# Attention with q and k handed over features first: rotary in that layout, one transpose of the maxima, rows placed by DMA

## The reference

```python
q_rot, k_rot = (rotate(q), rotate(k))        # x1*cos - x2*sin, x1*sin + x2*cos
scores = scale * np.matmul(q_rot, k_rot.transpose(0, 1, 3, 2))
scores = scores - np.max(scores, axis=-1, keepdims=True)
attn = np.exp(scores)
attn = attn / (np.sum(attn, axis=-1, keepdims=True) + 1e-09)
x = np.matmul(attn, v)                       # then heads side by side: 2304 x 512
h = x @ w_in;  x = (h - np.tanh(h)) @ w_out                          # layer 1
h = x @ w_in2; out = (h * (1 / (1 + np.exp(-1.702 * h)))) @ w_out2   # layer 2
```

## Time and profile before

| | us |
|---|---|
| median of 3 runs | 1189.93 (1188.15 to 1190.78) |
| the profiled execution | 1188.3, its span 1186.5 |
| start to the first score product | 21.0 |
| attention stage, 32 heads | 355.1 |
| the two layers and the end | 810.4 |
| TensorE busy, whole span | 1146.3 (97%) |
| granted TensorE clock | 1.000 throughout |

### The profile page before, as it was taken

One profiled execution on the slowest core, in us unless ns is written; L12 is line 12 of the kernel. 1 busy time (PEld: TensorE's weight loads), 2 busy tenths in 40 slices (PEclk: granted clock), 3 DMA queues, 4 the chain that ended last, 5 costly groups with the idle time before them and its releaser, 6 DMA issues.

```text
span 1186.5 us, 15852 instructions
## 1 busy us (share of the span) xinstructions
PE 1146.3 (97%) x6320; PEld 1051.4 (89%) x6320; DVE 471.2 (40%) x769; ACT 465.6 (39%) x811; POOL 188.9 (16%) x162
## 2 busy tenths in 40 slices
PE   5999999999999999999999999999999999999998
PEld 4788788777778999999999999999999999999997
DVE  6445545555553642333332323446332232323222
ACT  3655655665655532323222222345322222223222
POOL 6346545646501100000000000000000000000000
PEclk9999999999999999999999999999999999999999
DMA  4233344333321520000000000044000001000101
GB/s 112 51 86 79 78 117 138 86 101 91 104 64 56 186 81 27 27 28 27 27 28 27 1 28 27 27 134 133 27 27 22 5 27 28 27 27 1 27 1 27
DMA packets 78920, 65.79 MB, mean 55 GB/s; under 512 B 32256, under 2 KB 66048, under 8 KB 78848
## 3 DMA queue, kind: packets, MB, share of 16 engines
q1 hardware_dynamic: 78848, 64.79, 19.0%
HBM read 45.74 MB, written 14.23 MB: 51 GB/s over the span
## 4 chain that ended last, share of the span: by engine, by line
PE 89%; ACT 4%; DVE 4%; issue 2%; ACTq 0%; DVEq 0%
PE PS L556 34%; PE PS L574 17%; PE PS L571 17%; PE PS L515 10%; PE PS L500 4%; PE PS L503 3%; PE PS L478 3%; ACT k_hl L627 2%; ACT q_hh L633 1%; DVE q_lm L773 1%; DVE k_hl L768 1%; PE PS L467 1%; PE PS L487 1%; ACT q_lm L620 1%; DVE neg_max L762 1%
## 5 line engine op out<-in xcount | busy, mean ns | idle before, releaser
L556 PE MATMUL PS<-x_hi,w_parts 128*128 128x384 f32 x1536 | 423.1, 336 | 0.0
L556 PEld LDWEIGHTS PS<-x_hi,w_parts 128*128 128x128 f32 x1536 | 280.4, 188 | 4.3
L817 DVE TENSOR_TENSOR g_raw<-PS,act_t 128x384 f32<-128x384 f32 x192 | 107.1, 558 | 403.4 <-ACT act_t L688 202.7
L556 PE MATMUL PS<-x_lo,w_parts 128*128 128x384 f32 x768 | 257.2, 335 | 0.0
L571 PE MATMUL PS<-g_hi,w_parts 128*128 128x384 f32 x768 | 210.3, 334 | 0.8 <-DVE g_lo L822 0.8
L574 PE MATMUL PS<-w_parts,g_hi 128*128 128x512 f32 x576 | 195.1, 393 | 1.0 <-DVE y_sb L831 0.8
L515 PE MATMUL PS<-probs,v_one 128*128 128x288 f32 x640 | 181.7, 406 | 0.3 <-ACT pv_sb L616 0.3
L822 DVE TENSOR_TENSOR g_lo<-g_raw,g_hi 128x384 fp32r<-128x384 f32 x192 | 107.3, 559 | 113.6 <-ACT g_hi L695 113.6
L608 ACT ACTIVATE probs<-PS 128x576 f32<-128x576 f32 x160 | 104.2, 651 | 118.6 <-PE PS L503 113.8
L695 ACT ACTIVATE g_hi<-g_raw 128x384 fp32r<-128x384 f32 x192 | 100.8, 525 | 122.5 <-DVE g_raw L817 119.4
L762 DVE TENSOR_REDUCE neg_max<-PS 128x1 f32<-128x576 f32 x160 | 117.7, 754 | 76.9 <-PE PS L478 75.8
(11 more groups left out here) (64 smaller groups left out, 908.2 us busy)
## 6 DMA issues: line engine op xcount, KB each, us to landing
x_raw<-x_scratch SPq DMA_DIRECT2D x12, 768.0 KB, 4.5
raw_w<-moe_w_in_dram SPq DMA_DIRECT2D x32, 256.0 KB, 3.2
raw_w<-moe_w_out_dram SPq DMA_DIRECT2D x32, 256.0 KB, 3.4
k_h<-k_hl SPq DMA_DIRECT2D x16, 288.0 KB, 3.4
inv_wide<-inv_scratch SPq DMA_DIRECT2D x32, 144.0 KB, 3.0
x_scratch<-x_out SPq DMA_DIRECT2D x16, 288.0 KB, 2.4
x_scratch<-y_sb SPq DMA_DIRECT2D x6, 768.0 KB, 3.5
raw_k<-k_dram SPq DMA_DIRECT2D x16, 256.0 KB, 3.1
```

Of the source, the lines that this page charges most:

```text
L556: last = nc.tensor.matmul(h_banks[j % 2], w_parts[j][:, w, c * P:(c + 1) * P], x[par][:, c, :], start=(c == 0 and w == 0 and x is x_hi), s ...
L817: nc.vector.tensor_tensor(g_raw[:, j % 2, :], h_banks[j % 2], act_t[:, j % 2, :], ALU.subtract if m == 0 else ALU.mult).then_inc(g_done, 1)
```

## The change

The host hands over q and k with features first (64 x 576 per head), so that a pair is 128 rows, features of two heads. What follows in the kernel:

- `load` brings a pair's 128 x 576 block by one DMA into `raw`, and the same block again with each 32 rows swapped with their neighbours by four DMAs of 32 rows into `turned`. Rotary is then raw x cos + turned x sin, in place, three full-width operations. `raw` is now read by `keys_hi`, `queries_hi`, `keys_lo` and `queries_lo` directly, so that the next load into it waits for the low parts.
- `keys_across` and `queries_across` are gone, with their ring slots. `k_hl`, `q_hh`, `k_one` (before `k_h1`) and `q_max` (before `q_lm`) have four buffers, one per head; each head's parts are made three heads ahead (`PREPARED`).
- `maxima_across` is one transpose of a 128 x 5 tile. ACT copies the 5 x 128 result to `max_rows`, and SP places it in one row of `q_max` by two DMAs per head (`place_maxima`). The third and fourth matmul of a head's first score tile wait for that (`row_in`).
- The near scores of tiles 1 to 4 stand in the head before, two after each of its first two tiles; that of tile 0 stands a head earlier still, at its end.
- `copy_k` runs per head. `spread_inverse` is cut in two: `store_inverse` is SP's last step of an even head, `spread_inverse` follows the loads of the odd head.
- Positions keep their order, so that v is loaded plainly, and the result leaves by one DMA per unit, and one per tile at the very end.

```diff
-            if ahead and t < TILES - 1:
-                order.append(("M", h + 1, t))
-                if t == TILES - 2:
-                    order.append(("M", h + 1, t + 1))
-        if h % 2 == 0 and h + 2 < NHEADS:
-            order.append(("K", h + 2, 0))
-        if ahead:
-            order.append(("R", h + 1, 0))
+            if ahead and t < 2:
+                order += [("M", h + 1, 2 * t + 1), ("M", h + 1, 2 * t + 2)]
+            if ahead and t == 2:
+                order.append(("R", h + 1, 0))
         if h + 2 < NHEADS:
-            order.append(("Q", h + 2, 0))
+            order.append(("M", h + 2, 0))
+        turned = {t: [sb(f"turned_{t}{j}", [P, SEQ], stack=one_stack) for j in range(2)] for t in "qk"}
+        k_hl = [sb(f"k_hl{j}", [P, PADDED], F32R, one_stack) for j in range(4)]
+        k_one = [sb(f"k_one{j}", [P, PADDED], F32R, one_stack) for j in range(4)]
+        q_hh = [sb(f"q_hh{j}", [P, PADDED], F32R, one_stack) for j in range(4)]
+        q_max = [sb(f"q_max{j}", [P, SEQ], F32R, one_stack) for j in range(4)]
...
-                par = pair % 2
-                heads = src[2 * pair:2 * pair + 2, :, :]
-                sp.dma_start(raw[t][par][:, :, 0:FULL, :],
-                             heads[:, 0:FULL * P, :].rearrange("a (p i) d -> p a (i d)", i=FULL)).then_inc(loaded[t][par], 16)
-                sp.dma_start(raw[t][par][0:TAIL, :, FULL, :],
-                             heads[:, FULL * P:SEQ, :].rearrange("a p d -> p a d")).then_inc(loaded[t][par], 16)
+                par, first = pair % 2, pair * P
+                sp.dma_start(raw[t][par][:, :], src[first:first + P, :]).then_inc(loaded[t][par], 16)
+                for b in range(P // 32):
+                    to, of = slice(32 * b, 32 * b + 32), first + 32 * (b ^ 1)
+                    sp.dma_start(turned[t][par][to, :], src[of:of + 32, :]).then_inc(loaded[t][par], 16)
...
+            def copy_k(h):
+                sp.wait_ge(k_hi_done, h + 1)
+                sp.dma_start(k_one[h % 4][own(h % 2), 0:SEQ].bitcast(F32), k_hl[h % 4][own(h % 2), 0:SEQ].bitcast(F32)).then_inc(k_copied[h % 4], 16)
+
+            def place_maxima(h):
+                row = q_max[h % 4][one_row(h % 2), :].bitcast(F32)
+                sp.wait_ge(row_done, h + 1)
+                sp.dma_start(row[:, 0:FULL * P].rearrange("o (t n) -> o t n", t=FULL),
+                             max_rows[h % 2][0:FULL, :].bitcast(F32)).then_inc(row_in[h % 4], 16)
+                sp.dma_start(row[:, FULL * P:SEQ], max_rows[h % 2][FULL:TILES, 0:TAIL].bitcast(F32)).then_inc(row_in[h % 4], 16)
...
+            def store_inverse(pair):
+                sp.wait_ge(inv_done, pair + 1)
+                sp.dma_start(inv_scratch[pair].rearrange("a (p j) -> (a p) j", j=SEQ // HD), sums[pair % 2][:, :]).then_inc(inv_out, 16)
...
-            for h in range(NHEADS):
-                pair = h // 2
-                if h % 2 == 0:
-                    if pair + 2 < PAIRS:
-                        sp.wait_ge(k_roped, pair + 1)
-                        load("k", k_d, pair + 2)
-                        sp.wait_ge(q_roped, pair + 1)
-                        load("q", q_d, pair + 2)
-                    if h:
-                        fetch_sums(h - 1)
-                    if pair + 1 < PAIRS:
-                        load_v(pair + 1)
-                    if pair >= 2:
-                        store_x(pair - 2)
-                else:
-                    if pair + 1 < PAIRS:
-                        copy_k(pair + 1)
+            copy_k(1)
+            for h in range(-1, NHEADS):
+                pair = (h + 1) // 2
+                if h % 2 and pair + 2 < PAIRS:
+                    sp.wait_ge(k_lo_done, 2 * pair + 2)
+                    load("k", k_d, pair + 2)
+                    sp.wait_ge(q_lo_done, 2 * pair + 2)
+                    load("q", q_d, pair + 2)
+                if h % 2 and h >= 3:
+                    spread_inverse(h // 2 - 1)
+                if h >= 4 and h % 2 == 0:
+                    store_x(h // 2 - 2)
+                if h >= 1:
                     fetch_sums(h - 1)
-                    if pair:
-                        spread_inverse(pair - 1)
+                if h >= 0 and h % 2 == 0 and h // 2 + 1 < PAIRS:
+                    load_v(h // 2 + 1)
+                if h + 1 < NHEADS:
+                    place_maxima(h + 1)
+                if h + PREPARED < NHEADS:
+                    copy_k(h + PREPARED)
+                if h >= 2 and h % 2 == 0:
+                    store_inverse(h // 2 - 1)
...
-                store_tile((UNITS - 1) * UT + tile)
-            sp.wait_ge(y_stored, stored_by(LAYERS * UNITS))
+                row = (UNITS - 1) * UNIT + tile * P
+                sp.dma_start(out[row:row + P, :], y_sb[:, tile, :]).then_inc(y_stored, 16)
+            sp.wait_ge(y_stored, 16 * (n + UT))
...
+                par, at = pair % 2, ((pair - 1) * 2 + "kq".index(t)) * 2 + 1
+                pool.wait_ge(loaded[t][par], (pair // 2 + 1) * 80)
+                nc.gpsimd.tensor_tensor(turned[t][par][:, :], turned[t][par][:, :], sin_sb[:, :], ALU.mult).then_inc(pool_chain, 1)
+                nc.gpsimd.tensor_tensor(raw[t][par][:, :], raw[t][par][:, :], cos_sb[:, :], ALU.mult).then_inc(pool_chain, 1)
+                pool.wait_ge(pool_chain, at + 2)
+                nc.gpsimd.tensor_tensor(raw[t][par][:, :], raw[t][par][:, :], turned[t][par][:, :],
+                                        ALU.add).then_inc(k_roped if t == "k" else q_roped, 1)
 
...
-                slot = slot_columns(slot_of("R", h), PADDED)
-                for i in range(TILES):
-                    last = nc.tensor.transpose(slot[0:1, i * P:(i + 1) * P], neg_max[h % 2][:, i:i + 1], ident[:, :])
-                last.then_inc(r_ready, 1)
+                nc.tensor.transpose(slot_of("R", h)[0:TILES, 0, 0:P], neg_max[h % 2][:, :], ident[:, :]).then_inc(r_ready, 1)
...
+                    pe.wait_ge(k_copied[h % 4], h // 4 * 16 + 16)
+                slot = slot_halves(slot_of("S", h, t))
+                keys, rows = slice(t * P, (t + 1) * P), slice(0, HD + 1 if h % 2 == 0 else P)
+                for b in range(2):
+                    nc.tensor.matmul(slot[:, b, :], k_hl[h % 4][:, keys], q_hh[h % 4][:, b * HALF:(b + 1) * HALF],
+                                     start=True, stop=False)
+                if t == 0:
                     pe.wait_ge(q_lo_done, h + 1)
+                    pe.wait_ge(row_in[h % 4], h // 4 * 32 + 32)
                 for b in range(2):
+                    last = nc.tensor.matmul(slot[:, b, :], k_one[h % 4][rows, keys],
+                                            q_max[h % 4][rows, b * HALF:(b + 1) * HALF], start=False, stop=True)
...
-                    if ahead and t in (2, 3):
-                        near_scores(h + 1, t)
-                    if ahead and t == 3:
-                        near_scores(h + 1, 4)
-                    if t == 4 and h % 2 == 0 and h + 2 < NHEADS:
-                        keys_across((h + 2) // 2)
-                    if t == 4 and ahead:
-                        maxima_across(h + 1)
                     if now and g >= 0:
                         probs_v(g)
-                    if ahead and t in (0, 1):
-                        near_scores(h + 1, t)
+                    if ahead and t < 2:
+                        near_scores(h + 1, 2 * t + 1)
+                        near_scores(h + 1, 2 * t + 2)
+                    if ahead and t == 2:
+                        maxima_across(h + 1)
                 if h + 2 < NHEADS:
-                    queries_across(h + 2)
+                    near_scores(h + 2, 0)
...
+                if h >= 2:
+                    act.wait_ge(row_in[(h - 2) % 4], (h - 2) // 4 * 32 + 32)
+                nc.scalar.activation(max_rows[h % 2][0:TILES, :], slot_of("R", h)[0:TILES, 0, 0:P], ACT.Copy).then_inc(row_done, 1)
...
+                    if t == 2 and 0 <= h + 1 < NHEADS:
+                        row(h + 1)
                     if t == 2 and h in early_x:
                         cut_x(0, 0, 0, early_x[h])
-                    if t == 2 and h in early_w:
+                    if t == 3 and h in early_w:
                         cut_weights(0, early_w[h])
-                if h % 2 == 0 and h + 2 < NHEADS:
-                    keys_hi(h + 2)
-                if 0 <= h + 1 < NHEADS:
-                    row(h + 1)
-                if h % 2 == 0 and h + 2 < NHEADS:
-                    keys_hi(h + 3)
-                if h + 2 < NHEADS:
-                    queries_hi(h + 2)
+                    if h + PREPARED < NHEADS:
+                        if t == 3:
+                            keys_hi(h + PREPARED)
+                        if t == 4:
+                            queries_hi(h + PREPARED)
...
+            for h in range(-PREPARED, NHEADS):
+                for t in range(1, TILES):
                     if 0 <= h + 1 < NHEADS:
                         row_max(h + 1, t)
```

(18 more changed lines are left out.)

238 lines of the change are left out of this document (79 added, 159 removed).

## The result

The changed kernel takes 1207.51 us (median of 4 runs, 1204.84 to 1212.82) against 1189.87 (1188.15 to 1190.78): a ratio of 1.0156, 95% interval 1.0118 to 1.0193. It is slower by 17.6 us; 1201 had been forecast, in a range of 1176 to 1223. The profiled execution took 1208.82, its span is 1207.0. One of the four runs, 1212.82, had a mean granted clock of 0.933 where the other three had 0.981 to 0.984; it left no trace, and the interval on the median is some 4.5 us to either side.

What follows compares the result with a forecast made beforehand. TensorE bounds the kernel (busy 97%); SP's queue would lengthen pairs. 13.4 + 4.3 + 3 - 2 - 2.8 - 2.8 - 1.8 = +11.3 us: 1199.6 profiled, 1201 median, range 1176 to 1223.

Steps and rivals of the forecast that it cites:

- TensorE's work alone: Attention pair: transposes and a wait of 0.8 go, two transposes come back, 22.27 to 19.2 us.
- The chain through ACT and DVE: Odd head: near tile 2 waits 0.8 for DVE's maximum; head 9.8 to 10.1 us, pair 20.2 by this alone.
- SP's queue: Issues ahead of the even head's maxima make TensorE wait 3.9 us per pair; pair 23.4, +1.1.
- I take 0.60 plus the gap: SP's queue: assumed issue time of a 32-row load, 8 per pair, with no row for it; lower bound 0.43.
- rival (A): Cheap issues on SP: eight small loads at 0.45 to 0.48 each, pair 22.1, time 1183; chance 0.16.
- the prediction's own sign: SP's timeline after the change: turned loads issuing in under 0.5 would show the forecast of 0.6 each wrong.
- its clock is granted in full: TensorE before the change: clock read as 2.4 GHz in both layers and attention; no clock term in the sum.
- Weight issues at head 14: SP behind head 14: eight weight issues at 0.5 delay the next head's placement once, +4.3 us.
- The start: Before and in head 0: more issues, GpSimd passes and queries_hi(2); head 0 longer by 2, start 0 to 1.6 later, +3.
- Last heads: End of attention: no loads left in SP's queue, -2.8 us.
- End: End of kernel: three stores instead of six let the last be issued some 1.8 earlier, -1.8 us.
- The quoted rule that issuing is a small part of a transfer: Skill page on DMA issue, about 50 ns dispatch: queue would cost nothing, pair 20.2, time 1160; rival's chance 0.12.

Runs made afterwards that it cites:

- e7: Changed kernel with ten loads behind the placement, maximum and reciprocal ahead of the queries' low part, weight issues spread over heads 14 to 17: 1161.73 us.
- e8: e7 plus v's loads behind the placement in even heads and GpSimd's first rotary waiting for DVE's first low part: 1151.66 us.
- e5: Changed kernel with GpSimd's first rotary waiting until DVE has finished the first query's low part: 1203.99 us.
- e3: Changed kernel with one of k's four small turned loads cut in two from pair 2 on, same bytes: 1213.94 us.
- e1: Changed kernel with the ten loads of q and k in odd heads moved behind the maxima's placement and the keys' copy: 1185.04 us.

## Why the prediction came out right, and where it was wrong

The sign, the size within 7 us, and the place of the largest loss were right. The terms were less so.

1. **TensorE's work alone: 19.2 per pair. Too high.** The 19.2 that e7 and e8 take in heads 4 to 13 look like it, but hold waits in every odd head (0.4 to 1.4). Without a wait a head takes 8.95 (e8), a pair 17.9. The sum took the work of before as the pair's length less one wait of 0.8. In the even head of before TensorE also stands still twice between the first product with v and the second score tile, which from start to start take 1.08 and 0.82 there against 0.75 and 0.48 elsewhere (the second of these waits is a row of the timeline):

```profile
133.91 0.51 PE L500 MATMUL PS<-q_hh,k_hl 128*128 128x288 f32 x2 [0.33 <-DVE q_lm L773]
```

These 0.7 were not taken off; the other 0.6 I can't place. The forecast didn't hang on it, since the chain of point 2 was the longer one. The change does on TensorE what it says; without the queue it would have been faster than before.
2. **The chain through ACT and DVE: odd head 9.8 to 10.1, even head 9.0. Length right, waits not quite.** The odd heads of the changed kernel are 9.9 to 10.0, but for 19 (10.54) and 21 (10.17). In head 11 near tile 2 waits some 0.26 for DVE (155.89 to 156.90 for what takes 0.75 elsewhere) where 0.8 had been reckoned, and 0.5 stand ahead of it as a wait for the placement that had not. The even heads are 9.19 of work beside their wait, 0.2 more.
3. **SP's queue. Mechanism right, one term too large.** Reciprocal, loads, spread, sums and placements follow without a gap, as I had it. The step that failed is "I take 0.60 plus the gap" for a load of 32 rows: it measured 0.46 from start to start, the price of rival (A). I took the rows of loads of another shape over those of the earlier trace rows, which were nearer. The eight small loads took 1.5 less of the queue, and with them the wait is 2.47 in the mean of the ten even heads outside 14 and 16, not 3.9. By the prediction's own sign, turned loads issued in under 0.5, that was rival (A). The placement's landing, taken at 2.1, is 2.0 in the mean of these heads (1.8 to 2.4).
4. **What takes the place of the missing 1.4: the clock, not in the sum at all.** Seven of those ten heads run part of their work at the lower level, 1.6 us each, so 1.1 per pair. The sum had none of it; "its clock is granted in full" was read in the trace before and silently carried over into a kernel with idle time in it. The pair is 9.96 + 9.19 + 2.47 + 1.13 = 22.8, not 23.4; ten pairs of 0.5 more than the 22.27 of the earlier trace rows instead of 1.1 more. At full clock it would be 21.6, shorter than before: the price that rival (A) named was right, and its time of 1183 was missed by what it didn't hold, the clock, the weights and the start.
5. **Weight issues at head 14: +4.3 forecast.** Heads 14 to 17 take 57.8, which is 12.2 more than two pairs of 22.8. The eight issues were sized about right (5.25 us for 4.3), but not that 2 MB of weights move at the same time: the placement of head 16 lands 2.9 later than others, and its wait is 8.2 above the mean. The wait of head 14, 2.7 above it, comes from the load of `x_raw`, which wasn't in the sum at all: 1.7 more until the placement is issued (12.4 into the head instead of 10.7) and 1.2 more until it lands. Both heads at the lower clock make the rest. e7, which spreads the weight issues and changes the orders on SP and DVE, gives nearly all of it back.
6. **The start: +3 forecast, +9.2 measured.** Head 0 is 1.9 longer, as forecast (2); what failed is its start, 7.3 later and not 0 to 1.6. I priced DVE's and GpSimd's passes by the earlier trace rows, where DVE read PSUM, and let them run side by side. Both slow down when both read SBUF. e5 returns 5 us to the first score product, and half of that in the end, and part of the 7.3 varies between executions (28.35 here, 26.07 in e1). The rest wasn't taken apart: GpSimd's three passes per tensor, and the queues of loads in front of it.
7. **Last heads: -2.8 forecast, -0.9 measured.** Head 28 is 13.28 long still: it waits 2.46 for a row maximum, which stands on DVE behind a piece of the early weights (1.76) and the keys' low part (1.85), and the clock falls behind that wait too. Not tested by a run of its own.
8. **End: -1.8, measured -1.8. Layers: unchanged, right.** In both profiles they are 4326 matmuls, 803.37 and 803.39 us busy.
9. **The quoted rule that issuing is a small part of a transfer** would have put the pair at 20.2 and the kernel at 1160. The runs speak against it for this queue: an issue takes 0.35 to 0.67 us of SP, one issue more or less moves the placement by 0.45, and only a changed order came near 1160. The section quoted for the 50 ns describes DMAs that GpSimd issues, and this kernel issues all of its DMAs by SP; the figure should not have been held against these rows.

So the forecast was near in part by luck: what it had too large and what it lacked nearly cancel. Over heads 4 to 27 it overrated the waits of a regular pair by 17 us (12 x 1.4) and the handovers by 4; left out or underrated were the clock (12 x 1.13, 13.5), heads 14 to 17 (8), the start (6) and the last heads (2).

## What to carry to other kernels

Before a transfer that the critical engine waits for, count what is issued ahead of it on its queue, with the wait at the head of that row; then put the transfer first and the bulk loads behind it. The same holds for the in-order engine that releases the queue: here a row maximum and a reciprocal, 0.75 and 0.4 us, stood behind a part that nobody needs yet, and moving them ahead of it gave more (31 us) than moving the ten loads (22 us).

A wait on TensorE may cost more than its length, because the clock can fall behind it. A sum for a change that adds waits of 2 us and more needs that term; the rows at either clock, if there are any, give its size.

Where a change moves DVE's inputs from PSUM to SBUF, price its passes beside GpSimd, not alone.

## What the runs showed of the hardware

- In eight of the twelve even heads TensorE took 10.8 us for its 54 matmuls instead of 9.19, in head 14 11.35, with the granted clock at 0.5 for part of the head, behind waits of 2.18 us and more. In three it kept its clock, behind 2.14, 2.35 and 1.61; in e3 it kept it behind 2.66. No length of the wait separates the two kinds; what does stays open.
- A DVE pass over 576 columns with two inputs in SBUF takes 0.75 us alone and 1.8 to 1.95 beside GpSimd; GpSimd's goes from 1.4 to 1.9. From PSUM the keys' low part took 0.756 in the mean with GpSimd at work as much (188.9 us before, 182.6 after).
- SP issues a 32-row load of 72 KB in 0.42 us, 0.46 from start to start, a 128-row load of 288 KB in 0.42 in most places and up to 0.62, a placement of a row of maxima in 0.67 and 0.57. Why the loads of before took 0.59 and 0.64 wasn't tested.
- A placement (2.2 KB in two transfers) lands 2.0 us after the start of its second issue beside the loads of q and k, 3.2 beside the load of `x_raw`, and 4.8 beside the first weights.
